# A fused attention and two MoE layers: attention heads 0 to 5 folded two at a time, their halves added by VectorE

## What is computed

```
mask = q_bucket[:, :, :, None] == k_bucket[:, :, None, :]
scores = np.where(mask, scale * q @ k.T, -1e9)
attn = exp(scores - max) ; attn = attn / (sum + 1e-9)
x = (attn @ v), heads side by side            # 768 x 512
expert_idx = argmax(x @ w_gate)               # 8 experts, capacity 192
y = relu(x[rows of e] @ w1[e]) @ w2[e]        # 512 -> 1024 -> 512, times the gate weight
out = (h * tanh(softplus(h))) @ w_out,  h = y @ w_in   # 512 -> 2048 -> 512
```

## Time and profile before

| | |
|---|---|
| time, median of 3 runs | 399.43 us (398.72 to 400.5) |
| the profiled execution's own time | 399.76 us |
| its span | 397.6 us |
| attention loop | about 14 to 131 us of the span |

### The profile page before, as it was taken

The page is one execution under the profiler, slowest core; times in us unless marked ns, Lnnn a source line. Parts: engine busy times, 40 slices in busy tenths (PEclk is TensorE's granted clock), DMA queues, the critical chain, the costliest instruction groups (busy, mean ns, idle before and its releaser), DMA issues.

```text
span 397.6 us, 6821 instructions
## 1 busy us (share of the span) xinstructions
PE 387.2 (97%) x2423; PEld 350.2 (88%) x2424; DVE 283.4 (71%) x449; ACT 233.7 (59%) x448; POOL 100.0 (25%) x97
## 2 busy tenths in 40 slices
PE   8999999999999998999999999999999999999995
PEld 3689999999999797989998997989889998999984
DVE  4888988989988644550446636659899998877761
ACT  5969869859878333630435643556666656544531
POOL 1851321420700060029755325500000000000015
PEclk9999999999999999999999999999999999999999
DMA  8684933973910046996899999281000000000004
GB/s 287 221 199 111 266 78 101 300 170 91 407 61 2 2 160 250 381 362 225 294 336 385 312 389 347 99 277 42 2 0 0 2 0 2 0 0 2 0 5 158
DMA packets 16955, 62.89 MB, mean 158 GB/s; under 512 B 3088, under 2 KB 3984, under 8 KB 12448
## 3 DMA queue, kind: packets, MB, share of 16 engines
q1 hardware_dynamic: 15424, 58.61, 43.8%
q0 software_dynamic: 992, 3.19, 2.1%
q10 hardware_dynamic: 512, 0.73, 0.6%
HBM read 49.89 MB, written 3.19 MB: 134 GB/s over the span
## 4 chain that ended last, share of the span: by engine, by line
PE 57%; DMA 4%; POOL 1%; issue 1%; POOLq 0%; ACT 0%; DVE 0%; SPq 0%; ACTq 0%
PE ps L1002 17%; PE ps L1027 16%; PE ps L877 13%; PE ps L922 9%; DMA ring<-in_w 2%; PE ps L943 2%; DMA rows<-xg,sloti 1%; PE ps L903 1%; POOL rows L595 0%; POOLq L100 0%; POOL out L616 0%; DVE outs L1625 0%; ACT yh L1217 0%; ACT ysb L1211 0%; SPq L491 0%
## 5 line engine op out<-in xcount | busy, mean ns | idle before, releaser
L877 PE MATMUL ps<-xs,ring 128*128 x512 | 60.9, 277 | 0.7 <-DMA ring<-in_w 0.7
L877 PEld LDWEIGHTS ps<-xs,ring 128*128 128x128 f32 x512 | 59.3, 191 | 2.1 <-issue 1.7
L1152 ACT ACTIVATE pth<-ps 128x384 fp32r<-128x384 f32 x96 | 41.9, 490 | 20.2 <-PE ps L799 19.8
L1432 DVE TENSOR_TENSOR ptl<-ps,pth 128x384 fp32r<-128x384 f32 x96 | 48.9, 551 | 4.1 <-ACT pth L1152 3.2
L1375 DVE TENSOR_REDUCE nmax<-ps 128x1 f32<-128x768 f32 x48 | 45.6, 954 | 4.8 <-PE ps L680 2.5
L680 PE MATMUL ps<-ops 128*128 128x384 f32 x192 | 44.2, 352 | 0.1
L1109 ACT ACTIVATE prob<-ps,nmax 128x768 f32<-128x768 f32 x48 | 43.5, 906 | 0.1
L1002 PE MATMUL ps<-yh,wih 128*128 128x384 f32 x128 | 43.0, 336 | 0.3 <-ACT yh L1217 0.3
L1002 PE MATMUL ps<-yh,wlow 128*128 128x384 f32 x128 | 42.8, 335 | 0.0
L1521 DVE TENSOR_TENSOR w2lo<-ring,w2hi 128x1024 fp32r<-128x1024 f32 x28 | 38.1, 1361 | 6.6 <-ACT w2hi L1207 6.6
L1002 PE MATMUL ps<-yl,wih 128*128 128x384 f32 x128 | 41.9, 335 | 0.0
(11 more groups left out here) (185 smaller groups left out, 775.0 us busy)
## 6 DMA issues: line engine op xcount, KB each, us to landing
ring<-in_w SPq DMA_DIRECT2D x32, 1024.0 KB, 6.5
wraw<-in_w_in SPq DMA_DIRECT2D x11, 256.0 KB, 5.6
wraw<-in_w_out SPq DMA_DIRECT2D x11, 256.0 KB, 6.0
ops<-kh SPq DMA_DIRECT2D x12, 192.0 KB, 6.1
ops<-qh SPq DMA_DIRECT2D x6, 384.0 KB, 7.4
xg<-rows SPq DMA_DIRECT2D x1, 1539.0 KB, 7.0
raw<-in_vt SPq DMA_DIRECT2D x4, 384.0 KB, 5.3
wraw<-in_w_in SPq DMA_DIRECT2D x1, 1280.0 KB, 10.8
```

The source lines that it names most:

```text
L877: last = mm(ps[:, fc // 2, (fc % 2) * WIDE:(fc % 2) * WIDE + W], wa[:, 2 * fc // KF, kd, P * (fc % (KF // 2)):P * (fc % (KF // 2)) + P], x ...
L1152: av(pth[:, (n // HT) % 2, HT * b:HT * b + HT, n % HT, :], ps[:, tile_banks(n)[b], 0:HALF].rearrange("p (a c) -> p a c", c=P), ACT.Copy).t ...
L1432: V.tensor_tensor(ptl[:, m2, HT * b:HT * b + HT, u, :], ps[:, tile_banks(n)[b], 0:HALF].rearrange("p (a c) -> p a c", c=P), pth[:, m2, HT ...
```

## The change

Heads 0 to 5 go through the fold as three pairs. VectorE gets a new operation, `join(m)`, in turn 3m + 7 behind the row maximum, for m = 0 to 11: it adds partitions 64 to 127 of a half head's `ots` to partitions 0 to 63, and puts the sum into `ots[:, 0, half, :]`, in partitions 0 to 63 for an even head and 64 to 127 for an odd one. So one tile holds the sums of both heads of a pair. `fold_pair(k)` then folds one half (k % 2) of pair k // 2: three fp32 matmuls over 144 columns, namely a unit matrix of 128 and the gate weights of both heads in blocks. It is issued at the ends of turns 15, 20, 27, 32, 39 and 44. `scale_pair` scales it in the turn after, for both heads; inverse sums are taken once for a pair. The logits of heads 0 to 5 are gathered by halves and by even and odd head in a new tile, and GpSimd adds the two kinds in one more operation (`add_last_logits`). GpSimd's list is put in another order around these additions: the rounding of the keys is now a function of its own, `round_keys`, issued ahead of one of them. `evict` of an even head from 2 on waits for the half-fold that frees its tile, that of an odd one for a join. Heads 6 and 7 are folded as before.

```diff
+        FOLDS = {}
+        for g in range(PAIRED):
+            FOLDS[PER * g + 5 * HT], FOLDS[PER * g + 5 * HT + 5] = 2 * g, 2 * g + 1
+        FOLDS[2 * HT * (H - 2) + 3 * HT] = H - 2
+        assert STEPS == H - 2 and not any(("B", n) in TASKS for n in FOLDS)
         def fold_at(n):
-            h, other = divmod(n - 3 * HT, 2 * HT)
-            return h if h >= 0 and other == 0 else None
+            return FOLDS.get(n)
...
-            def add_logits(h):
-                hold(gp, s["passed_gp"], s["gm"], h + 1)
-                if h:
-                    hold(gp, s["passed_gp"], s["gt"], h)
+            def add_logits(k):
+                hold(gp, s["passed_gp"], s["gm"], k + 1)
+                if k:
+                    hold(gp, s["passed_gp"], s["gt"], k)
+                ts = slice(HT * (k % 2), HT * (k % 2) + HT)
+                nc.gpsimd.tensor_tensor(logits[:, ts, :, :].rearrange("p t h e -> p (t h e)"),
+                                        logits[:, ts, :, :].rearrange("p t h e -> p (t h e)"),
+                                        small["ex"][:, :, :].rearrange("p t e -> p (t e)"), ALU.add).then_inc(s["gt"], 1)
+            def add_last_logits():
+                hold(gp, s["passed_gp"], s["gt"], STEPS)
+                nc.gpsimd.tensor_tensor(small["lg"][:, :, :], logits[:, :, 0, :], logits[:, :, 1, :],
+                                        ALU.add).then_inc(s["gt"], 1)
+                hold(gp, s["passed_gp"], s["gm"], STEPS + 1)
+                hold(gp, s["passed_gp"], s["gt"], STEPS + 1)
                 nc.gpsimd.tensor_tensor(small["lg"][:, :, :], small["lg"][:, :, :], small["ex"][:, :, :],
...
             split_v(0)
+            round_keys(1)
             split_kq(1)
...
             for g in range(2, NPAIR):
+                round_keys(g)
+                if g > 2:
+                    add_logits(2 * g - 5)
                 split_kq(g)
-                add_logits(2 * g - 4)
                 gp.wait_ge(s["PV"], 2 + 4 * (g - 1))
                 split_v(g)
-                add_logits(2 * g - 3)
-            add_logits(H - 4)
+                add_logits(2 * g - 4)
+            add_logits(STEPS - 3)
...
+            def fold_pair(k):
+                if k == 0:
+                    pe.wait_ge(s["wg"], 16)
+                g, c = divmod(k, 2)
+                pe.wait_ge(s["os"], 4 * g + 2 + c + 1)
+                x_free()
+                for u in range(HT):
+                    last = mm(ps[:, XB, 2 * W72 * u:2 * W72 * u + 2 * W72], ots[:, 0, c, P * u:P * u + P],
+                              fold[:, 2 * W72 * g:2 * W72 * g + 2 * W72], start=True, stop=True)
+                last.then_inc(s["fw"], 1)
+                user[0] = ("fold", k, None)
             def fold_out(h, halves=(0, 1)):
-                if h == 0:
-                    pe.wait_ge(s["wg"], 16)
                 for half in halves:
...
                         last = mm(ps[:, XB, W72 * u:W72 * u + W72],
-                                  ots[:, h % 2, half, P * (u % HT):P * (u % HT) + P], fold[:, h, :],
+                                  ots[:, h % 2, half, P * (u % HT):P * (u % HT) + P], fold[:, W72 * h:W72 * h + W72],
                                   start=True, stop=True)
...
                 act.wait_ge(s["PV"], 2 + m + 1)
-                if m > 3:
-                    act.wait_ge(s["fw"], m // 2 - 1)
+                h, c = divmod(m, 2)
+                if h >= 2 and h % 2 == 0:
+                    act.wait_ge(s["fw"], h - 1 + c)
+                elif h >= 2:
+                    act.wait_ge(s["os"], 2 * h - 4 + c + 1)
                 av(ots[:, (m // 2) % 2, m % 2, :], ps[:, out_bank(m), 0:HALF], ACT.Copy).then_inc(s["OT"], 1)
...
-            def invert_sums(h):
-                cs = slice(NT * h, NT * h + NT)
-                dve.wait_ge(s["rc1"], h + 1)
+            def invert_sums(h, heads, done):
+                cs = slice(NT * h, NT * (h + heads))
+                dve.wait_ge(s["rc1"], h + heads)
                 V.reciprocal(rinv[:, cs], rinv[:, cs]).then_inc(s["rc"], 1)
-                dve.wait_ge(s["rc"], h + 1)
+                dve.wait_ge(s["rc"], done)
+            def join(m):
+                h, c = divmod(m, 2)
+                p = h % 2
+                dve.wait_ge(s["OT"], m + 2)
+                V.tensor_tensor(ots[D * p:D * p + D, 0, c, :], ots[0:D, p, c, :], ots[D:P, p, c, :],
+                                ALU.add).then_inc(s["os"], 1)
+            def scale_pair(k):
+                g, c = divmod(k, 2)
+                dve.wait_ge(s["fw"], k + 1)
+                x = ps[:, XB, 0:HT * 2 * W72].rearrange("p (t c) -> p t c", c=2 * W72)
+                r = rinv[:, 2 * NT * g:2 * NT * g + 2 * NT].rearrange(
+                    "p (h t) -> p t h", t=NT)[:, HT * c:HT * c + HT, :].unsqueeze(3)
+                if k:
+                    dve.wait_ge(s["gt"], k)
+                V.tensor_tensor(small["ex"].rearrange("p t e -> p (t e)").rearrange("p (t h e) -> p t h e", t=HT, h=2),
+                                x[:, :, 2 * D:2 * W72].rearrange("p t (h e) -> p t h e", h=2),
+                                r.to_broadcast([P, HT, 2, E]), ALU.mult).then_inc(s["gm"], 1)
+                V.tensor_tensor(xq[:, HT * c:HT * c + HT, 2 * g:2 * g + 2, :],
+                                x[:, :, 0:2 * D].rearrange("p t (h d) -> p t h d", h=2),
+                                r.to_broadcast([P, HT, 2, D]), ALU.mult).then_inc(s["fr"], 1)
...
                 r = rinv[:, NT * h:NT * h + NT].unsqueeze(2)
-                if 0 < h < H - 1:
+                if h < H - 1:
                     dve.wait_ge(s["gt"], h)
-                if h < H - 1:
                     V.tensor_tensor(small["ex"][:, :, :], x[:, :, D:W72], r.to_broadcast([P, NT, E]),
...
                     prepare("B", n - 1)
-                if fold_at(n - 1) is not None:
-                    invert_sums(fold_at(n - 1))
-                    scale_out(fold_at(n - 1))
+                k = fold_at(n - 1)
+                if k is not None and k < STEPS:
+                    if k % 2 == 0:
+                        invert_sums(k, 2, k // 2 + 1)
+                    scale_pair(k)
+                elif k is not None:
+                    invert_sums(k, 1, PAIRED + 1)
+                    scale_out(k)
                 if n + 2 < UNITS:
                     rowmax(n + 2)
+                m, other = divmod(n - 2 * HT - 1, HT)
+                if other == 0 and 0 <= m < 2 * STEPS:
+                    join(m)
                 prepare("A", n)
...
             projs[D * p:D * p + D, kq, at:at + n_bits] = inputs["proj"]
-    gate = np.tile(inputs["moe_w_gate"].reshape(H, D, E).transpose(1, 0, 2), (2, 1, 1))
-    same = np.tile(np.eye(D, dtype=np.float32)[:, None, :], (2, H, 1))
-    arrays = {"kt": kt, "qt": qt, "vt": vt, "first": first, "proj1": proj1, "projs": projs, "foldw": np.concatenate([same, gate], 2),
+    gate = inputs["moe_w_gate"].reshape(H, D, E)
+    same, none = np.eye(D, dtype=np.float32), np.zeros((D, E), np.float32)
+    wide = [np.block([[np.eye(P, dtype=np.float32), np.block([[gate[h], none], [none, gate[h + 1]]])]])
+            for h in range(0, H - 2, 2)]
+    foldw = np.concatenate(wide + [np.tile(np.block([[same, gate[h]]]), (2, 1)) for h in (H - 2, H - 1)], 1)
+    arrays = {"kt": kt, "qt": qt, "vt": vt, "first": first, "proj1": proj1, "projs": projs, "foldw": foldw,
               "w1": w1.reshape(E, DM // P, P, 2, F // 2).transpose(0, 3, 2, 1, 4),
```

More of the change, by code:

```diff
@@ L81, in attention_moe_mish @@
     W72 = D + E
+    PAIRED = NPAIR - 1
+    STEPS = 2 * PAIRED
     KF, KFF = F // P, FF // P
@@ L121, in c16 @@
             return cbs[:, b16_at[name][0]:b16_at[name][1]]
-        fold = place("fold", [P, H, W72], F32)
+        fold = place("fold", [P, H * W72], F32)
         projhi = place("projhi", [P, 2, P], F32R)
@@ L130, in attention_moe_mish @@
                   ("less", BF16))}
+        logits = place("logits", [P, NT, 2, E], F32)
         col = {n: place(n, [P, NT], F32) for n in
@@ L255, in attention_moe_mish @@
                   "pjh", "pjl", "wg",
-                  "S", "max", "P", "T", "hi", "lo", "PV", "OT", "xw", "fw", "fr", "pa", "pd", "vs", "rc", "tiny",
+                  "S", "max", "P", "T", "hi", "lo", "PV", "OT", "os", "xw", "fw", "fr", "pa", "pd", "vs", "rc", "tiny",
                   "g", "gex", "ohm", "lth", "gt", "gm", "gpos", "gst", "gkr", "hotr", "xga", "xgd", "perm", "tokc", "tokr", "si", "sc", "back", "wide", "xw0", "xw1", "xt", "xa", "xd",
@@ L422, in _ @@
             load_v(1)
-            sp.dma_start(fold[:, :, :], foldw).then_inc(s["wg"], 16)
+            sp.dma_start(fold[:, :], foldw).then_inc(s["wg"], 16)
             load_kq(2)
@@ L522, in split_v, with round_keys @@
                                         sub).then_inc(s["vs"], 1)
-            def split_kq(g):
-                rk = [raw[:, g % 2, n, :, :].rearrange("p t x -> p (t x)") for n in (1, 0)]
```

(23 more changed lines are left out.)

## The result

The changed kernel takes 401.52 us (median of 6 runs, 400.54 to 402.9) where the one before takes 399.08: ratio 1.0063, 95% interval 1.0041 to 1.0085, so 2.4 us slower. The forecast was slower, 403.0, range 399.4 to 405.4. The spans agree: the profiled one after has 399.3 us against 397.6.

A forecast was written before the change was run, and what follows sets the result against it. TensorE's weight-load queue was taken to set the attention loop's pace, with little room on VectorE. Joins 5.60 plus uncovered scaling 1.62, less 3.66 gained, made 3.6 us slower: 399.43 + 3.6 = 403.0, range 399.4 to 405.4.

The forecast's parts named there:

- TensorE's gain: Attention loop: six folds of 1.32 us become six half-folds of 0.71, so TensorE gains 3.66 us (3.5 to 3.9).
- turns 16, 27, 39: Sign to look for in the timeline: these turns 0.61 us shorter than before at the fold.
- The joins: Twelve VectorE additions between maximum and subtractions, 0.47 us each plus lost overlap, delay TensorE's next transposes: 5.60 us together.
- turns 16 to 19 and 28 to 31: Two joins per group beside km operations; VectorE's lag doesn't shrink, TensorE is 0.87 us late at each group's end.
- Turn 40: Join whose maximum starts a bit later after an eviction or a scaling: 0.62 us lost.
- The block by GpSimd: Joins of turns 10 and 22 wait for GpSimd's kl, lasting near 1.1 us; each turn loses 0.95 us.
- The join of turn 34: GpSimd's zeroing of yh and yl nearby blocks no join; did it block, this turn would lose up to 3 us.
- The lost overlap: VectorE loses 0.11 us at each change of partition range: 0.11 per even-head join, 0.22 per odd.
- Turns 9 and 21, the uncovered scaling: Without their folds, ScalarE's scaling of the next queries delays TensorE by 0.81 us in each, 1.62 together.
- Turn 33: Loses its fold but has no scaling of queries; ScalarE is ready in time, so no cost.
- The shift reaches the end: Behind the loop TensorE is nearly always busy, so the loop's 3.6 us shift carries to the kernel's end.

The follow-up runs named there:

- the hold: The changed kernel, but GpSimd starts kl of the second and third pair only after the join of turn 10 or 22: ratio 1.0028 to the kernel before.

## Why the prediction was right, and where it was not

- **TensorE's gain.** Right: 3.66 forecast; six folds of 1.32 went, and six half-folds of 0.71 to 0.74 came, which leaves 3.5 to 3.6. (The prediction's "turns 16, 27, 39" should read 15, 27, 39.)
- **The joins.** Right in mechanism, and in sum: 5.60 forecast; 0.20 + 0.85 + 0.68 + 0.85 + 0.68 + 0.37 + 0.48 + 0.78 = 4.9 by the turns. The kernel without joins has a loop 4.7 shorter. Nearly each term was 0.1 too large, those of turns 16 to 19 and 28 to 31 by 0.2: TensorE does wait 0.15 for the second subtraction, but the turn gets that time back. Turn 40 was too small, 0.62 for 0.78: turn 39 is 0.6 shorter now, so the inverse sums begin at T - 0.40 and not at T - 1.02, the scaling follows after a wait of 0.26, and the maximum starts at T + 0.68 and not at T + 0.37. What the 0.26 is was not looked into.
- **The block by GpSimd.** Right: durations of 1.07 and 1.09 forecast as 1.1; the hold took 1.0 us away. The join of turn 34 kept its 0.55 (from 103.45) beside the memset of `yh` (101.59 to 104.94), as forecast.
- **The lost overlap.** Right, 0.03 instead of -0.08, at the places named.
- **Turns 9 and 21, the uncovered scaling.** The sum was right (1.62 against 0.72 + 0.79), and for turn 21 the cause. For turn 9 it was half of it. The subtraction is through at 39.97, T + 2.73 as forecast, but the scores, held until qo has landed, end their weight loads only at 40.02, so either alone would bring the next T, 40.03, to about where it is. The step that failed is that a turn without its fold has nothing to cover but the scaling: taking the scaling out of turn 9 leaves it at 3.03.

```profile
39.40 0.94 PE L708 MATMUL ps<-ops 128*128 128x384 f32 x4 [0.47 <-DMA ops<-qo]
```
```profile
39.42 1.02 DVE L1505 TENSOR_TENSOR ptl<-ps,pth 128x384 fp32r<-128x384 f32 x2 [0.85 <-ACT pth L1194]
```

- **Turn 33.** Costed at nothing, it paid 0.14 the same way. The weight loads name no releaser here, but GpSimd's first memset waits for the same landing, and begins when they do:

```profile
101.45 0.65 PEld L708 LDWEIGHTS ps<-ops 128*128 128x128 f32 x4 [0.20 <-issue]
```
```profile
101.45 0.10 POOL L604 MEMSET mark<- 128x1 f32 x1 [1.13 <-DMA ops<-qo]
```

- **The way to the end.** "The shift reaches the end" was too firm. The loop is 3.0 us longer (3.6 forecast), the time 2.4 with an interval of 1.6 to 3.4. The first pair of traces shows 1.3 us less behind the loop, the second only 0.5, and the two traces of the kernel before differ by 0.8 there. Over all traces whose work behind the loop is unchanged, that stretch is 267.8 to 268.6 in the three with whole folds and 266.6 to 268.4 (mean 267.4) in the eight with half-folds. Execution explains a part; whether another is the change's is open.

## What to carry to other kernels

Where two engines alternate within a turn, an operation costs what it exceeds the slack of its place in the turn, not its share of the idle time; and work that is taken off the bounding engine was covering waits, so ask what is late next (here ScalarE's scaling and a DMA's landing ate half the gain). A fold made half as long for TensorE left VectorE's scaling behind it as long as it was. If the same change is wanted, move the added operations into turns in which the bounding engine has more to do, and not into the last ones before a busy stretch: with the joins moved, the scaling moved and the wait split, the same folds were 0.28% faster than the kernel before, where they had been 0.63% slower.

## What the runs showed of the hardware

- A VectorE addition with two SBUF inputs waits for a GpSimd subtraction between SBUF tensors that runs: 0.55 became 0.68 to 1.87 us, and each such join ended 0.41 or 0.42 after the subtraction did. Where GpSimd had a second subtraction to do (2.13 for 1.84), the join got in between the two. The maximum, which reads PSUM, kept its 0.95 beside the same subtraction, and a join kept 0.55 beside a memset.
- The joins' two inputs in different partition ranges cost no throughput (0.55 us, as with both in one range), but 0.11 us of overlap at their start, and 0.11 more behind them where the output changed range.
